# An attention kernel whose last value products of a pair are spread over three steps instead of two

## The reference

```python
scores = scale * np.matmul(q, k.transpose(0, 1, 3, 2))      # B, H, S, D = 4, 8, 576, 64
h = np.maximum(x @ w1 + b1, 0.0)                            # x from the distances of positions
scores = scores + (h @ w2).transpose(2, 0, 1)[None]
scores = scores - np.max(scores, axis=-1, keepdims=True)
attn = np.exp(scores)
attn = attn / (np.sum(attn, axis=-1, keepdims=True) + 1e-09)
attn_out = np.matmul(attn, v)
x = attn_out.transpose(0, 2, 1, 3).reshape(2304, 512)
out = ((1.0 / (1.0 + np.exp(-(x @ w_gate)))) * (x @ w_val)) @ w_out
```

## Time and profile before

| | |
|---|---|
| time, three runs | 756.55 us median, 756.42 to 757.21 |
| the profiled execution | 755.89 us, its span 754.1 us |
| granted TensorE clock, mean | 0.995 of full |
| load of q and k, issue to landing | 4.9 us median, 3.9 to 4.9 in all but one, 8.8 in that of pair 10 |
| PE busy | 718.0 us (95% of the span) |
| DVE busy | 509.5 us (68%) |
| ACT busy | 456.4 us (61%) |
| POOL busy | 358.9 us (48%) |
| chain that ended last | PE 70%, DVE 11%, issue 7%, ACT 7% |
| of it in `values`, L1184 | 6% |

### The profile page before, as it was taken

The page is one execution under the profiler, slowest core; times in us unless marked ns, Lnnn a source line. Parts: engine busy times, 40 slices in busy tenths (PEclk is TensorE's granted clock), DMA queues, the critical chain, the costliest instruction groups (busy, mean ns, idle before and its releaser), DMA issues.

```text
span 754.1 us, 14209 instructions
## 1 busy us (share of the span) xinstructions
PE 718.0 (95%) x4944; PEld 588.1 (78%) x4944; DVE 509.5 (68%) x1066; ACT 456.4 (61%) x923; POOL 358.9 (48%) x482
## 2 busy tenths in 40 slices
PE   6778899999989999999999999999999999999998
PEld 3335676676657666679888998999899899989996
DVE  5997777777757777756951787586078768714851
ACT  5997777777757676758633763474277536625720
POOL 0002555555558898975646544464056165604500
PEclk9999999999999999999999999999999999999999
DMA  4887133222262232113330224121012421201102
GB/s 136 213 209 173 41 81 103 71 73 66 69 201 75 78 102 66 33 52 121 114 111 3 82 67 158 56 85 56 0 57 76 148 84 57 84 0 41 45 9 76
DMA packets 56598, 63.64 MB, mean 84 GB/s; under 512 B 22096, under 2 KB 47824, under 8 KB 56528
## 3 DMA queue, kind: packets, MB, share of 16 engines
q1 hardware_dynamic: 56096, 62.65, 27.7%
q10 hardware_dynamic: 432, 0.09, 0.1%
HBM read 42.67 MB, written 9.44 MB: 69 GB/s over the span
## 4 chain that ended last, share of the span: by engine, by line
PE 70%; DVE 11%; issue 7%; ACT 7%; DMA 2%; POOL 2%; SPq 1%; ACTq 0%; DVEq 0%; POOLq 0%
PE f_ps L1277 20%; PE z_ps L1222 19%; PE y_ps L1222 9%; DVE feats L876 7%; PE v_ps L1184 6%; PE x_ps L1222 5%; ACT probs L713 4%; PE so_ps L1130 4%; PE ty_ps L1141 2%; PE tx_ps L1151 2%; ACT pt L707 2%; DVE sum_eps L916 1%; DVE neg_scores L901 1%; DMA qk_whole<-in_qk 1%; PE so_ps L1125 1%
## 5 line engine op out<-in xcount | busy, mean ns | idle before, releaser
L1222 PE MATMUL z_ps<-xc,wc 128*128 128x384 f32 x864 | 165.5, 336 | 0.7 <-DVE wc L951 0.5
L544 POOL TENSOR_SCALAR probs<-probs,recip 128x512 f32<-128x512 f32 x128 | 88.5, 692 | 147.9 <-DVE recip L921 147.9
L1222 PEld LDWEIGHTS z_ps<-xc,wc 128*128 128x128 f32 x864 | 150.5, 188 | 4.5 <-ACT keep L740 1.7
L713 ACT ACTIVATE probs<-neg_scores,neg_max 128x576 f32<-128x576 f32 x144 | 110.9, 770 | 62.5 <-DVE neg_max L901 62.4
L901 DVE CUSTOM_DVE_ANT_0 neg_scores<-so_ps,bias 128x576 f32<-128x576 f32 x128 | 91.9, 755 | 4.5 <-PE so_ps L1113 3.2
L570 POOL TENSOR_TENSOR wc<-t_raw,wc 128x512 fp32r<-128x512 f32 x37 | 48.8, 1318 | 87.6 <-ACT wc L732 87.6
L1222 PE MATMUL y_ps<-xc,wc 128*128 128x384 f32 x432 | 86.6, 334 | 0.5 <-DVE sig L967 0.5
L1277 PE MATMUL f_ps<-wo_h,h_h 128*128 128x512 f32 x216 | 84.4, 391 | 0.7 <-issue 0.7
L740 ACT ACTIVATE keep<-z_ps 128x384 f32<-128x384 f32 x108 | 52.9, 490 | 52.0 <-PE z_ps L1222 51.3
L1277 PE MATMUL f_ps<-wo_h,h_l 128*128 128x512 f32 x216 | 84.4, 391 | 0.0
L1277 PE MATMUL f_ps<-wo_l,h_h 128*128 128x512 f32 x216 | 84.2, 390 | 0.0
(11 more groups left out here) (113 smaller groups left out, 1456.2 us busy)
## 6 DMA issues: line engine op xcount, KB each, us to landing
qk_whole<-in_qk SPq DMA_DIRECT2D x16, 608.0 KB, 4.9
w_stage<-in_w_gate SPq DMA_DIRECT2D x18, 512.0 KB, 3.6
w_stage<-in_w_val SPq DMA_DIRECT2D x18, 512.0 KB, 3.6
bias<-bias_rows SPq DMA_DIRECT2D x12, 576.0 KB, 5.1
out<-out_sb SPq DMA_DIRECT2D x18, 256.0 KB, 2.0
v_main<-in_v SPq DMA_DIRECT2D x32, 128.0 KB, 2.3
x_whole<-attn_transposed SPq DMA_DIRECT2D x9, 384.0 KB, 5.6
wo_whole<-in_w_out SPq DMA_DIRECT2D x6, 512.0 KB, 4.5
```

The costliest lines, as they stand in the source:

```text
L544: nc.gpsimd.tensor_scalar(row[:, 0:NT * P], row[:, 0:NT * P], by, 1.0, ALU.mult, ALU.mult).then_inc(normed, 1)
L713: nc.scalar.activation(probs[s % RING][:, place, :], neg_scores[:, place, :], ACT.Exp, bias=neg_max[:, stat(s, place)], scale=-1.0, accum_ ...
L1222: last = nc.tensor.matmul(quad_ps[bank][n % 2][:, 0:CH], wc[:, n % 2, wl, W_PARTS.index(wp), t, :], xc[:, X_PARTS.index(x), xl, t, :], sta ...
```

## The change

The last 320 queries' values (g = 1) are computed in three portions, in m2 (tiles 0, 1), m3 (tiles 2, 3) and R (tile 4), where it was m2 (tiles 0, 1, 2) and m3 (tiles 3, 4). In R the portion stands between the step's scores and the transposes. ACT's copy of these sums, which was the first instruction of R, becomes the last one of R, behind the exponential. For the last pair, whose R would be behind the end of the loop, tile 4 follows directly on tiles 2 and 3 in the last drain step. The signal `valued`, which comes with tile 4, moves with it. Nothing else is edited: neither the instructions themselves nor their number.

```diff
--- before.py
+++ after.py
@@ -304,7 +304,7 @@
             W_TASKS[71 + n] = piece
         EARLY = {STEPS - 1: ("P1", "P2"), STEPS: ("P6", "P5"), STEPS + 1: ("P7",)}
 
-        VALUE_SLOTS = {0: (0, (0, 1, 2)), 1: (0, (3, 4)), 2: (1, (0, 1, 2)), 3: (1, (3, 4))}
+        VALUE_SLOTS = {0: (0, (0, 1, 2)), 1: (0, (3, 4)), 2: (1, (0, 1)), 3: (1, (2, 3)), R: (1, (4,))}
 
 
         ident, ident_swap = ident_wide[:, 0:P], ident_wide[:, REM:REM + P]
@@ -750,8 +750,6 @@
             for s in range(STEPS + DRAIN):
                 pair, m = divmod(s, SPP)
                 units = units_of(s) if s < STEPS else ()
-                if m == 4 and pair >= 1:
-                    copy_values(pair - 1)
                 if m in QK_STEPS and pair + 1 < PAIRS:
                     high_qk(pair + 1, QK_STEPS.index(m))
                 if m != R:
@@ -761,6 +759,8 @@
                     move_a(s - LAG)
                 for u, place in units if m == R else units[1:]:
                     exponentials(s, u, place)
+                if m == R and pair >= 1:
+                    copy_values(pair - 1)
                 if s == STEPS - 1:
                     high_w(1, "B1")
                     keep_sum(0, "P1")
@@ -1240,6 +1240,8 @@
                         nc.tensor.matmul(v_ps[:, 0:P + REM], ident, ident_wide[:, :], start=True, stop=True)
                 if m == 1 and pair >= 1:
                     values(pair - 1, *VALUE_SLOTS[m])
+                if m == R and pair >= 1:
+                    values(pair - 1, *VALUE_SLOTS[m])
                 if 0 <= c < STEPS and c % SPP == R:
                     transpose_r(c)
                 elif 0 <= c < STEPS:
@@ -1247,6 +1249,8 @@
                     transpose_a(c)
                 if m in (0, 2, 3) and pair >= 1:
                     values(pair - 1, *VALUE_SLOTS[m])
+                if s == STEPS + 3:
+                    values(pair - 1, *VALUE_SLOTS[R])
                 for name in EARLY.get(s, ()):
                     product(0, name)
```

## The result

The changed kernel takes 763.63 us (median of 5, 763.18 to 764.03) against 757.21 us for the kernel before (5 runs, 756.42 to 759.39). The ratio of the times is 1.0081, 95% interval 1.0063 to 1.0098: it is slower, clear of noise. The profiled execution took 763.63, its span is 761.8, at a mean granted clock of 0.993.

The account below looks back on a forecast made before the run. TensorE was taken to bound m2, m3 and R, ScalarE and VectorE alternating in m0 and m1. Terms 2.1 + 1.05 + 1.1 + 1.9 + 0.84 = 7.0 on 756.55 gave 763.5, range 757.5 to 767.

Parts of the forecast that it names:

- Ordinary pairs: Pairs 1 to 8: R starts 0.54 earlier, its transposes end 0.84 later than that, net +0.30; 2.1 for seven.
- The copy: Copy of the sums, moved behind exp of R: covered by ScalarE's wait there; up to 0.42 a pair if uncovered.
- SyncE's queue: In R(8), loads queued behind the wait for the values land 1.05 later: +1.05 (bounds 0 and 1.8); ordinary pairs covered.
- R(9): R step of pair 9, behind the stall, where TensorE's tiles run slower: +1.1 (bounds 0.5 and 1.5).
- R(15): R step of pair 15: chain is TensorE alone, m2 gives nothing: +0.84 (0.54 to 1.0).
- R(10) to R(14): VectorE holds R's start, so m2's gain is 0.18 in all; less slacks the five cost 1.9 (bounds 0.3 and 3).
- No surcharge: Rival: a tile costs 0.54 wherever it is, pairs 1 to 8 are even; +2.8, 759.3; chance 0.17.
- The hidden tile: Rival: the tile in R doesn't delay the move, exp of R up to 0.54 earlier in eight pairs; 752.2; chance 0.08.
- Late loads: Rival: q and k land late in ordinary pairs, some 0.5 in each of 13; +6.5 on top, 770; chance 0.07.
- The even case: Rival: delays of R run into slack, VectorE's small operations fall differently late; sum near 0.5, 757; chance 0.13.

Follow-up runs that it names:

- the run with the old portions late: Changed kernel, but from the values of pair 8 on in the old portions of 3 and 2 tiles: 760.81, ratio 1.0042.
- the small multiplications: Kernel before, one small multiplication added between R's scores and transposes: 760.79 with weights of 128 by 64, 758.96 with 128 by 128.
- the run with two buffers: Changed kernel with tile 4 behind R's transposes, load of v behind q and k, two buffers for tile 4's probabilities: 753.12, ratio 0.9944.

## Why the prediction was right

**The time.** Forecast +7.0 and 763.5, measured 763.63 against a median of 757.21 in the later runs, so +6.4. Direction and size hold, and so does the mechanism in the ordinary pairs, in the queue and in the last R. In the traces the stages from R(0) to the end of the span add up to 6.99. Much of that closeness is luck, as the late pairs show below.

**Ordinary pairs: right.** "Net +0.30" a pair was measured as 0.30 (period 15.98 to 16.28), +2.09 for seven, against 2.1. Both parts show: 0.54 less in m2, 0.84 more in R. The drain that the Trainium skill's page "TensorEngine Tiling (Array Packing)", section Tiling Modes, states for a change of mode agrees with 0.26 and 0.59 against 0.17 and 0.44 in the pair of runs that differ in the shape alone.

**The copy: right.** Cost 0 in ordinary pairs, shown by two runs.

**SyncE's queue: right in kind, low in size.** In terms of R(8)'s scores the forecast had the load 1.59 later (1.05 and the 0.54 by which R starts earlier); it was 2.16. The wait for the values gave 1.68 of it. The rest, 0.48, came in SyncE's own issues, where the store took 1.03 instead of 0.56. ScalarE's wait for q and k grew by 1.27 (6.03 against 4.76), where I had given 0.75 as a sign. I had also counted nine loads in that queue; there are six, behind four of v. Loads in ordinary pairs did not become late: the load of q and k starts at 131.85 and, with the longest ordinary landing of 4.9, is there at 136.8; the next m2 asks for it at 137.7 (1.36 behind its scores at 136.33, as before).

**R(9): the wrong place.** I put 1.1 there, as the tile would run at the slow rate. It ran at the full one, in 0.69, and R(9) to R(10) is even (16.80 against 16.84). TensorE had stood 4.77 for the long wait, and 2.98 before; the mean granted clock of 222 to 231 is 0.81 in both kernels, and in 228 to 230 of the changed one it is 0.50, the lower level of 1.2 GHz. That slow stretch fell on m3: in the chains of waits its first transposes behind the wait took 1.08 instead of 0.63 and its portion 2.13 instead of 1.96, while R(9)'s scores, slow before at 1.74, took 0.99. In the place of the 1.1 stands the 0.74 that is lost between ScalarE's wait and R(9). From R(8) to R(10) the change cost 2.80, where my terms gave 1.59 and 1.1, 2.7.

**R(15): right.** 0.87 against 0.84.

**R(10) to R(14): right in the sum, by luck.** 1.72 against 1.9 in the traces. The delay at R is as forecast: the move is last again (its wait grew to 1.40, from 0.24 to 0.40), and in pair 10 the exponential starts 3.52 behind R's scores instead of 2.96, 0.56 later where my term had 0.57. But my terms carried nearly all of it on to the next pair, some 0.4 in each, and the traces don't: the five are +0.09, +0.70, -0.10, +0.20 and +0.83. The two large ones hold something that was not in my sum, a small operation of VectorE that takes long. Between R(11) and R(12) it took 1.16 where it had taken 0.70, and between R(14) and R(15) 2.04 (the last section shows it), where none had taken over 0.76:

```profile
275.57 1.16 DVE L916 TENSOR_SCALAR sum_eps<-row_sum 128x2 f32<-128x2 f32 x1 [1.21 <-ACT probs L713]
```

How these fall together isn't the change's: R(14) to R(15) is 17.44 in the profile of the kernel before, 17.49 in the run with the old portions late, and 18.69 to 18.72 in five other runs with the old order there. The two runs with the load of v moved, which differ by the change alone, show 86.28 - 85.87 = 0.41 for the five pairs together. So what I had wrong is how much of the delay at a late R reaches the next pair; which slack took up the rest stays open. The run with the old portions late gives 2.8 for all of this and R(15), against my 2.7, but 1.2 of it may be of this kind; the two runs with the load of v moved give 1.1 for the same stages (513.95 against 512.84). So 1.1 to 2.8 is what the late part is shown to cost.

**The rivals.** No surcharge is refuted by the small multiplications. The hidden tile is refuted as I put it (ahead of the transposes nothing hides it), and behind them it needs a second buffer. Late loads did not come. The even case lived on slack in the late pairs. There was more of it than I took, but it could not cover what the ordinary pairs, the queue and R(15) cost.

## What to carry to other kernels

Moving work between steps of one engine pays only where that engine, and not another, sets the start of the step it leaves; and it costs in full where another engine waits for what it is put in front of. Before moving an instruction behind others, list who must wait until its inputs may be overwritten: here a buffer's reuse, hidden by the old order, cost 3.4 (756.55 against 753.12). And a signal that moves takes its queue with it: ask which transfers stand behind the wait, in the one step where the queue is long above all.

## What the runs showed of the hardware that I had not expected

VectorE's smallest operation can take as long as two of GpSimd's long ones. In the changed kernel, R(14)'s pair (the timeline, with R's move first):

```profile
318.58 0.70 ACT L707 ACTIVATE pt<-tx_ps 128x640 f32<-128x640 f32 x1 [1.40 <-PE tx_ps L1154]
...
323.22 1.00 POOL L608 TENSOR_TENSOR xc<-x_stage,xc 128x384 fp32r<-128x384 f32 x1
...
323.42 2.04 DVE L916 TENSOR_SCALAR sum_eps<-row_sum 128x2 f32<-128x2 f32 x1 [1.00 <-ACT probs L713]
...
324.18 1.26 POOL L570 TENSOR_TENSOR wc<-t_raw,wc 128x512 fp32r<-128x512 f32 x1
...
325.50 0.17 DVE L921 RECIPROCAL recip<-sum_eps 128x2 f32<-128x2 f32 x1
...
325.77 0.69 POOL L544 TENSOR_SCALAR probs<-probs,recip 128x512 f32<-128x512 f32 x1 [0.33 <-DVE recip L921]
```

The operation on 128 by 2 elements normally takes 0.17. Here it takes 2.04 and ends with the second of two tensor-by-tensor operations of GpSimd (324.18 + 1.26), though nothing in the program makes it wait for them. It took 0.77 at the same point in the run with two buffers and 2.43 in the kernel before with the load of v moved, by how the two engines' work fell together; in that last run it had even started, at 313.81, before the first of the two, at 313.96. That is the one us and more by which the late pairs differ among kernels with the same instructions. The Trainium skill's "GPSIMD Engine Reference", section Specifications, says that GpSimd shares its interfaces to SBUF, the on-chip memory, with VectorE, with contention for VectorE's instructions in a 2-port mode or with two inputs in SBUF. The trace agrees in that the operations end together, 325.46 and 325.44; no run shows in which mode VectorE's ran. That the shared interface is the cause is argued, not shown, since no run took one of the two operations away.

A change of weight shape and back, between instructions with weights of 128 by 128, cost 0.24: 0.09 ahead and 0.15 behind. That is more than the 0.17 that a small multiplication cost by itself.
